# Second mixture: order of the small steps around its tiles, on VectorE, ScalarE, SyncE and GpSimd

## The reference

```python
# 1. sparse attention: 8 heads of 64; keys within 15 positions, plus one max-pooled key
#    (value: the mean) per block of 32; softmax over both sets -> x (1536, 512)
# 2. first mixture, dense: 4 experts, F = 1024
for e in range(4):
    out += p[:, e:e+1] * (np.maximum(x @ w1[e], 0) @ w2[e])
# 3. second mixture, sparse: 8 experts, F = 1024
skip_score = x @ w_skip
do_compute = skip_score > 0
out = x.copy()
xc = x[do_compute]
logits = xc @ w_gate
e_idx = np.argmax(logits, axis=1)               # one expert for each token
probs = softmax(logits); gate_w = probs[chosen expert]
y[mask] = gate_w[mask] * (np.maximum(xc[mask] @ w1[e], 0.0) @ w2[e])     # for each expert e
out[do_compute] = xc + y
```

## Time and profile before

| | us |
|---|---|
| median of three runs | 783.56 |
| profiled execution, its own time | 782.77 |
| its span, first to last instruction | 780.9 |
| PE busy | 733.6 (94%) |
| VectorE busy | 288.4 (37%) |
| ScalarE busy | 205.6 (26%) |
| POOL busy | 71.3 (9%) |
| share of PE in the chain that ended last | 88% |

### The profile page before, as it was taken

One profiled execution on the slowest core, in us unless ns is written; L12 is line 12 of the kernel. 1 busy time (PEld: TensorE's weight loads), 2 busy tenths in 40 slices (PEclk: granted clock), 3 DMA queues, 4 the chain that ended last, 5 costly groups with the idle time before them and its releaser, 6 DMA issues.

```text
span 780.9 us, 12635 instructions
## 1 busy us (share of the span) xinstructions
PE 733.6 (94%) x4610; PEld 605.1 (77%) x4611; DVE 288.4 (37%) x824; ACT 205.6 (26%) x498; POOL 71.3 (9%) x100
## 2 busy tenths in 40 slices
PE   5689999999999999999999999999999965899995
PEld 4488897989898998989989899898989832444442
DVE  4977673532441221343212143313232353431431
ACT  3753552532230110222102031120202002431330
POOL 2521000000000000000000000001010123132222
PEclk9999999999999999999999999999999988999998
DMA  9892821213330000033000011020202857997000
GB/s 208 198 219 62 170 59 31 49 25 108 108 108 1 1 0 0 0 108 107 0 0 0 0 41 67 1 81 1 81 1 81 325 197 283 396 396 295 21 3 21
DMA packets 77093, 75.24 MB, mean 96 GB/s; under 512 B 54232, under 2 KB 54508, under 8 KB 76656
## 3 DMA queue, kind: packets, MB, share of 16 engines
q1 hardware_dynamic: 74080, 69.72, 28.5%
q0 software_dynamic: 2800, 4.66, 1.9%
q10 hardware_dynamic: 160, 0.20, 0.1%
HBM read 67.22 MB, written 8.24 MB: 97 GB/s over the span
## 4 chain that ended last, share of the span: by engine, by line
PE 88%; DVE 3%; DMA 2%; issue 2%; ACT 1%; ACTq 1%; DVEq 1%; POOL 1%; POOLq 0%; SPq 0%
PE ps L1232 23%; PE ps L1234 23%; PE ps L1233 23%; PE ps L1519 6%; PE ps L1497 5%; PE ps L1294 1%; PE ps L1266 1%; PE ps L1417 1%; PE ps L1280 1%; DMA acc<-stage 1%; PE ps L1245 1%; PE ps L1407 1%; DVE acc L886 1%; PE ps L1479 1%; DMA acc<-in_moe_w 1%
## 5 line engine op out<-in xcount | busy, mean ns | idle before, releaser
L1232 PE MATMUL ps<-xt_hi,w_hi 128*128 128x384 f32 (+1 forms) x508 | 172.9, 340 | 0.0
L1234 PE MATMUL ps<-xt_hi,w_lo 128*128 128x384 f32 (+1 forms) x508 | 170.1, 335 | 0.0
L1233 PE MATMUL ps<-xt_lo,w_hi 128*128 128x384 f32 (+1 forms) x508 | 170.0, 335 | 0.0
L697 ACT ACTIVATE h_hi<-ps 128x384 fp32r<-128x384 f32 x128 | 63.0, 492 | 359.3 <-PE ps L1234 359.1
L1232 PE MATMUL ps<-w_hi,h_hi 128*128 128x512 f32 x384 | 151.7, 395 | 0.0
L1234 PE MATMUL ps<-w_hi,h_lo 128*128 128x512 f32 x384 | 149.9, 390 | 0.0
L1233 PE MATMUL ps<-w_lo,h_hi 128*128 128x512 f32 x384 | 149.8, 390 | 0.0
L932 DVE SCALAR_TENSOR_TENSOR h_lo<-ps,h_hi 128x384 fp32r<-128x384 f32 x128 | 71.2, 556 | 167.3 <-ACT h_hi L697 167.2
L1232 PEld LDWEIGHTS ps<-xt_hi,w_hi 128*128 128x128 f32 x508 | 95.4, 188 | 1.5 <-issue 0.8
L1233 PEld LDWEIGHTS ps<-xt_lo,w_hi 128*128 128x128 f32 x508 | 95.5, 188 | 0.5
L1234 PEld LDWEIGHTS ps<-xt_hi,w_lo 128*128 128x128 f32 x508 | 95.4, 188 | 0.0
(11 more groups left out here) (173 smaller groups left out, 598.1 us busy)
## 6 DMA issues: line engine op xcount, KB each, us to landing
sets<-in_moe_w SPq DMA_DIRECT2D x64, 512.0 KB, 7.4
stage<-in_moe_w SPq DMA_DIRECT2D x24, 512.0 KB, 3.8
stage<-in_k SPq DMA_DIRECT2D x16, 192.0 KB, 4.2
acc<-in_v SPq DMA_DIRECT2D x4, 768.0 KB, 6.4
x_rows<-acc SPq DMA_DIRECT2D x4, 768.0 KB, 4.1
out_rows<-acc SPq DMA_DIRECT2D x4, 768.0 KB, 5.6
acc<-in_moe_w POOLq DMA_DIRECT2D x4, 512.0 KB, 4.5
acc<-in_moe_w SPq DMA_DIRECT2D x4, 512.0 KB, 5.3
```

The source lines that it names most:

```text
L697: nc.scalar.activation(h_hi[:, f, :], ps[:, f % 2, 0:GT], ACT.Relu).then_inc(h_hi_ok, 1)
L1232: mm(dst, a_hi, b_hi, start=start, stop=False)
L1233: mm(dst, a_hi, b_lo, start=False, stop=False)
L1234: return mm(dst, a_lo, b_hi, start=False, stop=stop)
```

## The change

- The columns `id_of` and `gate_of` are widened so that every tile has its own; the loops around the written-out turns go, tile numbers become constants.
- SP: `store` is cut in two. Of the last group, the rows for `x1_rows` go ahead of the last three pieces of set 1; `set_ready` for set 1 is raised without the wait for a gather; the rows for the output go after the gather of tile 0, and two pieces of set 2 right behind them.
- POOL waits for the scatter before, then for `add_x`; the marks (`hold`) go; the gathers of the last three turns go.
- ScalarE: numbers of set and place are loaded two tiles ahead; the layer 1 copies of a change stand right after `relu_h`, the layer 2 copies after `copy_ht`.
- VectorE: in a turn, `add_x(i)`, layer 2 weights, `make_ids(i+6)`, two register loads, and then, inside the `If` for the next tile, `copy_x(i+2)`, layer 1 weights, `rows_in(i+3)`. Ahead of the loop the weights of set 1 are copied before the list arrives, and three ids instead of six are made ahead of `copy_x(1)`.
- `choose` reads the logits out of PSUM and needs one copy less.
- PE's `layer2` waits for `y_ok`, and the last `next_rows` goes.

```diff
 SP
+            load_set(1, 1, range(1))
+            keep(G - 1)                       # rows to x1_rows
+            load_set(1, 1, range(1, PIECES))
+            arrived(1, 0)
+            sp.wait_ge(gathered[0], 16)
+            send_out(G - 1)                   # rows to the output
+            load_set(2, 0, range(2))
+            arrived(1, 1)
             sp.wait_ge(gathered[1], 16)
-            arrived(1, 0)
-            load_set(2, 0)
-            arrived(1, 1)
+            load_set(2, 0, range(2, PIECES))
             load_set(2, 1)
 POOL
+            def turn(i):
+                gp.wait_ge(scattered, 16 * i)
+                gp.wait_ge(y_ok, i + 3)
+                scatter_rows(i % SLOTS, ids(i))
+                if i + 1 < TILES:
+                    with gp.If(tiles > i + SLOTS - 3):
+                        gp.wait_ge(id_ok, i + SLOTS - 1)
+                        gather_rows((i + SLOTS - 1) % SLOTS, ids(i + SLOTS - 1))
+                    with gp.If(tiles > i + 1):
+                        turn(i + 1)
 ScalarE
+            def turn(i, ago, now, then, at_now, at_then):
+                relu_h(i)
+                with act.If(now < then):
+                    place(then, at_then, 0)
+                copy_ht(i)
+                with act.If(ago < now):
+                    act.wait_ge(r2_done, i)
+                    place(now, at_now, 1)
+                beyond, at_beyond = set_at(i + 2), waits_at(i + 2)
+                ...
 VectorE, ahead of the loop
+            first, second, at_second = set_at(0), set_at(1), waits_at(1)
+            with dve.If(first < second):
+                dve.wait_ge(r1_done, 1)
+                place(second, at_second, 0)
             dve.wait_ge(list_in, 16 * SIDES)
-            for i in range(1, SLOTS + 1):
+            for i in range(1, AHEAD + 1):
                 make_ids(i, i)
+            copy_x(1)
             dve.wait_ge(r2_done, 1)
...
 VectorE, a turn
+            def turn(i, ago, now, then, at_now, at_then):
+                add_x(i, i)
+                with dve.If(ago < now):
+                    place(now, at_now, 1)
+                make_ids(i + SLOTS, i + SLOTS)
+                beyond, at_beyond = set_at(i + 3), waits_at(i + 3)
+                if i + 1 < TILES:
+                    with dve.If(tiles > i + 1):
                         copy_x(i + 2)
-                        now, then, beyond = set_at(i), set_at(i + 1), set_at(i + 2)
-                        with dve.If(then < beyond):
-                            place(i + 1, beyond, 0)
-                        add_x(i, at)
-                        rows_in(at + 3, TURNS // SLOTS * r + 1 + (at + 3) // SLOTS)
                         with dve.If(now < then):
-                            place(i, then, 1)
-                        make_ids(i + SLOTS, at + SLOTS)
+                            dve.wait_ge(r1_done, i + 2)
+                            place(then, at_then, 0)
+                        rows_in(i + 3, 1 + (i + 3) // SLOTS)
+                        turn(i + 1, now, then, beyond, at_then, at_beyond)
 PE
             def layer2(done, now):
+                pe.wait_ge(y_ok, done)
                 pe.wait_ge(ht_ok, done)
...
-            next_rows(tiles + 1)
             layer2(tiles + 1, E2 - 1)
```

More of the change, by code:

```diff
@@ L595, in _ @@
             gather_rows(SLOTS - 1, ids(SLOTS - 1))
[L596 to L604, removed]
-                        gp.wait_ge(id_ok, i + SLOTS - 1)
[L606 to L610, removed]
+            def turn(i):
[4 more added lines that the diff above has]
+                    with gp.If(tiles > i + SLOTS - 3):
+                        gp.wait_ge(id_ok, i + SLOTS - 1)
+                        gather_rows((i + SLOTS - 1) % SLOTS, ids(i + SLOTS - 1))
+                    with gp.If(tiles > i + 1):
+                        turn(i + 1)
+            turn(1)
         @block.scalar
@@ L802, in _ @@
             tiles = act.value_load(table[0:1, 0:1], min_val=1, max_val=TILES)
[L803 to L829, removed]
+            first, second, at_second = set_at(0), set_at(1), waits_at(1)
+            with act.If(first < second):
+                place(second, at_second, 0)
+            third, at_third = set_at(2), waits_at(2)
+            def turn(i, ago, now, then, at_now, at_then):
[8 more added lines that the diff above has]
+                if i + 1 < TILES:
+                    with act.If(tiles > i + 1):
+                        turn(i + 1, now, then, beyond, at_then, at_beyond)
+            turn(1, first, second, third, at_second, at_third)
         @block.vector
@@ L835, in _ @@
             dve.sem_inc(acc_ok, 2)
-            dve.sem_inc(y_ok, 1)
+            dve.sem_inc(y_ok, 2)
             dve.sem_inc(rows_ok, 2)
@@ L1176, in set_at, with waits_at, place @@
                 return dve.value_load(table[0:1, bass.ds(i + SET_OF, 1)], min_val=0, max_val=E2 - 1)
[L1178 to L1181 removed]
+            def waits_at(i):
+                return dve.value_load(table[0:1, bass.ds(i + WAIT_OF, 1)], min_val=0, max_val=AHEAD)
+            def place(then, at, layer):
                 dve.wait_ge(set_ready, 2 * then + 1 + layer)
@@ L1189, in _ @@
             tiles = dve.value_load(table[0:1, 0:1], min_val=1, max_val=TILES)
+            first, second, at_second = set_at(0), set_at(1), waits_at(1)
+            with dve.If(first < second):
+                dve.wait_ge(r1_done, 1)
+                place(second, at_second, 0)
             dve.wait_ge(list_in, 16 * SIDES)
-            for i in range(1, SLOTS + 1):
+            for i in range(1, AHEAD + 1):
                 make_ids(i, i)
-            now, then = set_at(0), set_at(1)
-            with dve.If(now < then):
-                place(0, then, 0)
+            copy_x(1)
             dve.wait_ge(r2_done, 1)
@@ new lines, in _ @@
+            with dve.If(second < third):
+                dve.wait_ge(r1_done, 2)
+                place(third, at_third, 0)
+            with dve.If(first < second):
+                place(second, at_second, 1)
+            rows_in(3, 1)
+            for i in range(AHEAD + 2, SLOTS + 1):
+                make_ids(i, i)
+            fourth, at_fourth = set_at(3), waits_at(3)
+            def turn(i, ago, now, then, at_now, at_then):
[4 more added lines that the diff above has]
+                beyond, at_beyond = set_at(i + 3), waits_at(i + 3)
+                if i + 1 < TILES:
+                    with dve.If(tiles > i + 1):
+                        copy_x(i + 2)
+                        with dve.If(now < then):
+                            dve.wait_ge(r1_done, i + 2)
+                            place(then, at_then, 0)
+                        rows_in(i + 3, 1 + (i + 3) // SLOTS)
+                        turn(i + 1, now, then, beyond, at_then, at_beyond)
@@ L1226, in _ @@
+            turn(1, second, third, fourth, at_third, at_fourth)
         @block.tensor
```

70 lines of the change are left out of this document (29 added, 41 removed).

## The result

The kernel after takes 814.33 us (median of 4, 812.8 to 815.4) against 783.82 us for the kernel before in the same comparison: ratio 1.0387, interval 1.0366 to 1.0408, +30.5 us. The forecast was +17.1 us, 801, and its range ended at 813. The direction was right, the size 13.4 us too small, and the range too short by 1.3 us.

A forecast was written before the change was run, and what follows sets the result against it. The prediction took PE to bound the second mixture, so waits between layer 2 and the next layer 1 are paid in full. 33.5 - 5.4 - 9.7 - 1.3 = +17.1 us on the 783.56 median: 801 us, range 793 to 813.

The forecast's parts named there:

- VectorE's turn: Tiles 3 to 13: copy_x falls behind the end of layer 2, after add_x, ids and loads, delaying layer 1: +33.5 us.
- Rival 3: VectorE's sequencer runs ids and loads past add_x's wait, before layer 2 ends: 783.5 us, not slower; chance 0.06.
- ScalarE's stalls: Layer 1 of tiles 3, 4, 10, 11 no longer waits for ScalarE's weight copies: -5.4 us.
- the end: After the last scatter, without POOL's extra gather, the closing drain ends earlier: -1.3 us.
- The waits that I had costed at nothing: Queue waits: PE on y_ok 0, POOL on the scatter no change, hold 0 to 0.1 us at the last scatter.
- The clock: PE's granted clock in the new gaps ahead of layer 1: no loss in the forecast.
- the seam: Start of the second mixture, up to layer 1 of tile 2: earlier gathers and weights, -9.7 us.
- rival 1: PE's clock falls in the new gaps: four tiles, 1.9 us each, 808 us; all eleven, 822; chance 0.18.
- rival 2: At the start, entries and list lose to moved traffic: gain 5.7 instead of 9.7 us, 805 us; chance 0.1.
- The set stream itself is not late: Weight sets arrive in time, since from tile 3 on tiles are spaced wider than before; no cost given.

The follow-up runs named there:

- Copies first: Kernel after, with copy_x(i+2) and the layer 1 weights ahead of add_x(i) again in VectorE's turn, ids and register loads at its end: 776.01 us, ratio 0.9916.
- ScalarE's part alone: Kernel before with only ScalarE's changes: numbers a tile ahead, layer 1 copies right after relu_h, layer 2 copies after copy_ht: 777.79 us, ratio 0.9942.
- the order alone: Kernel before with only VectorE's order turned: add_x, layer 2 weights and ids ahead of copy_x, loads at the turn's head: 821.62 us, ratio 1.0494.
- numbers late: Kernel after, with ids and two register loads moved behind copy_x, layer 1 weights and rows_in; add_x still ahead: 794.49 us, ratio 1.0162.
- quiet seam: Copies first, with SP's output rows and first two pieces of set 2 held until the gather of tile 1 has landed: 780.98 us, ratio 0.9971.
- the seam of before: Copies first, with SP's issues in the order of the kernel before, only the marks for set 1 staying early: 777.32 us, ratio 0.9932.
- fill the seam: Copies first, with SP resuming once the list is read back and 28 filler matmuls on PE behind layer 2 of tile 0: 773.0 us, ratio 0.9866.
- fillers in the gap: Kernel after, with ten filler matmuls on spare data on PE behind every turn_h: 806.97 us, ratio to before 1.0315.

## Why the prediction was right in direction and short in size

*VectorE's turn: right*, 33.7 against 33.5. By kind: tiles without change 2.9, 2.6, 2.6 and 2.5 (2.4 forecast), with layer 2 weights 2.9 and 2.9 (3.0), layer 1 weights 3.1 (3.1), both 3.5, 3.5, 3.8 and 3.5 (3.7). That the sum agrees to 0.2 is in part luck: the tiles without change came 1.0 us dearer in all than forecast, those with both copies 0.6 cheaper. What carried it is that the sequencer's loads were counted, though they are not among the busy instructions: two of the chain's loads (L1178 at 716.8, L1181 at 717.4) begin 0.6 us apart, as forecast. "Copies first" shows the term from the other side: with `copy_x` back under layer 2 it is zero.

*Rival 3 (the sequencer runs past the wait of `add_x`): not so.* The id's load (L1163, 715.90) begins after `add_x` (715.69) and not ahead of it.

*ScalarE's stalls and the end: right*, -5.4 and -1.3; "ScalarE's part alone" shows the first by itself. The waits that I had costed at nothing (PE on `y_ok`, POOL on the scatter, `hold`) leave no remainder in the sum.

*The clock: the step that failed.* Of the 14.8 us by which the sum was short (31.9 against 17.1), 10.2 are the clock and 4.4 the seam. I had set the forecast at no loss, and put rival 1 at 0.18, because the gaps of up to 3.65 us are nearer to an idle that held the clock (1.98) than to one that did not (6.74). Between two rows so far apart a distance is no evidence; the runs put the fall into the middle of the new gaps. In the kernel after, idle of 3.00 to 3.76 us ahead of layer 1 was followed by 0.50 in all five tiles that had it (3, 4, 9, 10, 11), 2.47 to 2.50 in none of three, and 2.84 to 2.86 in one of three. Tiles 5 and 6 have the same idle, 2.84, and came out differently, so its length alone does not decide. The other runs widen the open band: the clock fell after 2.27 us in "copies first" (tile 3), after 2.47 in "the order alone" (tile 9) and after 2.74 in two of three tiles of "numbers late". No run tells what decides there. Rival 1 had the mechanism and the price (1.9 a tile, measured 1.70), and named four tiles where it was six: its 808, two more tiles (3.4) and the seam's missing 4.4 are 816, against 814.3. The chances took rivals 1 and 2 as alternatives, but both came; with four tiles the two together would have been 812, inside the range, and the two further tiles took it over the end. The Trainium skill (TensorE: Matmul & The Clock Gate, HAM oscillation) tells of a loop that starts each tile at the lower clock; the trace agrees for six tiles of eleven, where the lower clock came about a microsecond into layer 1, and shows that the loop is not closed, since layer 1 ends each time at 1.00 again and five tiles in between never fell.

*The seam: the right sign, mis-sized*, 5.3 for 9.7, which is rival 2's figure (5.7). From the last logits on, the gather of tile 0 came 1.5 us earlier (1.6 forecast) and layer 1 of tile 0 0.9 (1.3). Then the list lost: the chain of the kernel after has the entries' landing

```profile
636.18 5.12 DMA route_list<-entry,slot
```

and the chain of the kernel before has

```profile
638.93 2.17 DMA route_list<-entry,slot
```

2.95 us more, where I had given back 1: the output rows (634.04) and the two pieces behind them were on the queues by then. The last entries were issued 1.0 us sooner after the last logits, so the list is issued 1.9 us later and the gather of tile 1 starts 2.05 us later, not 0.35 earlier. The quiet seam, without that traffic, has the list 3.1 us sooner than "copies first" has it with the traffic: rival 2 had the cause, at the entries alone. And the list holds more than that gather: ScalarE stands in the wait for the entries and issues the list before its `relu_h(0)`, so that layer 2 of tile 0 starts late, and at 0.50 (5.57 us where it takes 3.67): layer 1 of tile 1 is 2.2 us earlier, not 6.4. In the prediction the list was a matter of POOL's gathers only; that it stands ahead of a step of PE's on ScalarE was not seen.

*"The set stream itself is not late": true of the kernel after, and only because it is slow.* "Copies first", the quiet seam, the seam of before and "fill the seam" wait for it.

*What stays open*: why 2.84 us of idle did not let the clock fall in one tile and did in the next; and what of the entries' 5.12 us is the output rows' and what the weights'. The experiments at the seam moved both together.

## What to carry to other kernels

Between a release (here U) and the instruction that the bound engine waits for, count everything that the in-order engine issues, register loads and ids too, here some 0.6 us from one load to the next: an early load helps only where it is early for its engine, behind the urgent step and not ahead of it. Where PE is the bound, an idle gap that repeats is paid twice where the clock falls, and the forecast needs a row of a gap of that length, or a range that holds both outcomes. When a stage is made tighter, ask for the next supply (here the weight stream): of two gains made at the seam (the quiet seam, the fillers there) each was handed back to it within three tiles.

## What the runs showed of the hardware

- In these gaps the granted clock fell not in the idle but behind it: 1.00 in the idle stretch, 0.50 with PE at work a microsecond later, and 1.00 again before the layer ended. Each of the six took 5.35 us.
- Ten small matmuls (1.79 us) in a gap that stayed as long as it was kept the clock in five tiles of the six; the sixth was left with 2.13 us of idle.
- The last indirect write of the entries landed after 5.12 us with output rows and two pieces of weights issued 2 us ahead of it (5.33 and 5.17 in "fillers in the gap" and "numbers late", which have the same order), and after 2.17 us in the kernel before, where the weights of set 2 were issued only at 648.57 (2.29, 2.10 and 2.10 in "ScalarE's part alone", "the order alone" and "fill the seam").
- Two executions of an unchanged attention stage differ by 1.7 us, as much as the smallest terms here; spans are better compared from a step that both kernels share.
